# One core, attention and two feed-forward layers: state products of both streams in turns, weight splits of the first tile one step later, duo 0 begun by stream

## The reference

```python
for t in range(S):
    kt, vt, rt, wt = (k[:, :, t], v[:, :, t], r[:, :, t], w[:, :, t])
    cur = np.einsum('bhd,bhe->bhde', u[None] * kt, vt)
    y[:, :, t] = np.einsum('bhd,bhde->bhe', rt, state + cur)
    state = wt[:, :, :, None] * state + np.einsum('bhd,bhe->bhde', kt, vt)
```

## Time and profile before

| | |
|---|---|
| median of 3 runs | 1038.68 us (1038.28 to 1040.86) |
| the profiled execution | 1039.2 us |
| its span, first to last instruction | 1037.2 us |
| PE busy | 1011.8 us (98%) |
| DVE, ACT, POOL busy | 559.3, 289.1, 31.5 us |
| mean granted TensorE clock | 0.997 |

### The profile page before, as it was taken

One profiled execution on the slowest core, in us unless ns is written; L12 is line 12 of the kernel. 1 busy time (PEld: TensorE's weight loads), 2 busy tenths in 40 slices (PEclk: granted clock), 3 DMA queues, 4 the chain that ended last, 5 costly groups with the idle time before them and its releaser, 6 DMA issues.

```text
span 1037.2 us, 29081 instructions
## 1 busy us (share of the span) xinstructions
PE 1011.8 (98%) x12448; PEld 986.6 (95%) x12448; DVE 559.3 (54%) x1170; ACT 289.1 (28%) x604; POOL 31.5 (3%) x29
## 2 busy tenths in 40 slices
PE   4899999999999999999999999999999999999998
PEld 4789999999999999999999999999999999999998
DVE  6576575654655655646542345655455545455454
ACT  3424424224133142241222333222222222222211
POOL 3600100000000000000000000000000000000000
PEclk9989999999999999999999999999999999999999
DMA  7453231301212113011010222110101010101000
GB/s 181 110 147 106 54 101 29 89 25 33 86 52 63 29 52 90 2 52 37 24 48 13 84 84 85 39 46 1 46 1 46 2 45 0 45 0 46 1 24 23
DMA packets 42167, 53.01 MB, mean 51 GB/s; under 512 B 5184, under 2 KB 42048, under 8 KB 42048
## 3 DMA queue, kind: packets, MB, share of 16 engines
q1 hardware_dynamic: 40624, 51.04, 17.3%
q10 hardware_dynamic: 1424, 0.23, 0.2%
HBM read 39.46 MB, written 9.44 MB: 47 GB/s over the span
## 4 chain that ended last, share of the span: by engine, by line
PE 95%; DMA 2%; DVE 1%; issue 1%; SPq 1%; ACT 0%; DVEq 0%; ACTq 0%
PE products L164 17%; PE products L165 16%; PE products L166 16%; PE acc L164 11%; PE acc L166 11%; PE acc L165 11%; PE products L688 6%; PE products L745 2%; PE products L732 1%; PE products L703 1%; DMA w_v<-in_w_dram 1%; PE products L717 1%; PE products L665 1%; DMA stage<-in_w_a_dram 0%; SPq L360 0%
## 5 line engine op out<-in xcount | busy, mean ns | idle before, releaser
L164 PE MATMUL products<-x_parts,weights_hi 128*128 128x384 f32 x576 | 201.4, 350 | 3.1 <-DMA x_parts<-f_y 1.3
L165 PE MATMUL products<-x_parts,weights_hi 128*128 128x384 f32 x576 | 194.6, 338 | 0.0
L166 PE MATMUL products<-x_parts,weights_lo 128*128 128x384 f32 x576 | 194.3, 337 | 0.0
L1207 DVE TENSOR_SCALAR leaky_low<-products,leaky_al 128x384 f32<-128x384 f32 x128 | 79.0, 617 | 169.4 <-PE products L166 169.3
L1067 DVE TENSOR_TENSOR g_sb<-a_g,products 128x384 f32<-128x384 f32 x96 | 53.2, 554 | 203.2 <-issue 141.5
L1154 ACT ACTIVATE leaky_g_hi<-leaky_g_sb 128x384 fp32r<-128x384 f32 x128 | 67.3, 525 | 295.0 <-DVE leaky_g_sb L1212 295.0
L510 ACT ACTIVATE g_hi<-g_sb 128x384 fp32r<-128x384 f32 x96 | 50.3, 524 | 247.0 <-DVE g_sb L1067 247.0
L164 PEld LDWEIGHTS products<-x_parts,weights_hi 128*128 128x128 f32 x576 | 108.5, 188 | 8.1 <-issue 4.6
L165 PEld LDWEIGHTS products<-x_parts,weights_hi 128*128 128x128 f32 x576 | 108.6, 189 | 0.0
L166 PEld LDWEIGHTS products<-x_parts,weights_lo 128*128 128x128 f32 x576 | 108.6, 188 | 0.0
L164 PE MATMUL acc<-g_hi,weights_hi 128*128 128x384 f32 x288 | 97.8, 340 | 2.4 <-DVE g_lo L1073 2.4
(11 more groups left out here) (86 smaller groups left out, 1784.5 us busy)
## 6 DMA issues: line engine op xcount, KB each, us to landing
k_in<-in_k_dram SPq DMA_DIRECT2D x16, 336.0 KB, 4.1
r_in<-in_r_dram SPq DMA_DIRECT2D x16, 336.0 KB, 5.6
stage<-in_w_out_dram SPq DMA_DIRECT2D x14, 384.0 KB, 3.2
w_v<-in_v_dram SPq DMA_DIRECT2D x16, 288.0 KB, 3.2
y_dram<-x_in SPq DMA_DIRECT2D x8, 576.0 KB, 3.0
x_in<-y_dram SPq DMA_DIRECT2D x8, 576.0 KB, 4.5
out_dram<-leaky_out_sb SPq DMA_DIRECT2D x7, 576.0 KB, 3.3
stage<-in_w_dram SPq DMA_DIRECT2D x10, 336.0 KB, 3.9
```

Source lines behind the costliest of these rows:

```text
L164: pe.matmul(out, w_hi, x_hi, start=first, stop=False)
L165: pe.matmul(out, w_hi, x_lo, start=False, stop=False)
L166: return pe.matmul(out, w_lo, x_hi, start=False, stop=last)
L1207: dve.tensor_scalar(self.low[f % 2][:, :], h, 0.0, self.al[:, f:f + 1], ALU.min, ALU.mult).then_inc(self.low_ready, 1)
```

## The change

1. `outputs`: in duos 1 to 7 the weighted values of stream 1 come first, and then the state products of both streams, block by block in turns, uncrossed and then crossed. Before, stream 0's came around the weighted values, then all of stream 1's. Duo 0 keeps one stream after the other.
2. Weights of tile 0: pieces 6 to 10, 12 and 14 are split one step later (`FIRST_NEW`), and ACT does so behind `g_hi` and not ahead of it. Piece 3 is split between the outputs of the two streams of duo 0.
3. Duo 0: the leaf of stream 1 goes into `acc`; PE makes leaf and level 1 of stream 0, then leaf and level 1 of stream 1; DVE steps stream 0's keys for level 2 ahead of stream 1's first step. SP waits for the second `w` before it issues the first three pieces.
4. Duo 1: its `w` is loaded from ACT's queue between the outputs of duo 0, as soon as the weighted values have read `v`, and not from SP's behind the moves; the first steps of its keys and queries stand ahead of step 0 of tile 0 and not in it.

```diff
-HI_AT = [2, 3, 4, 9, 11, 11]
+HI_AT = [2, 3, 4, BEFORE_TILES, 11, 11]
+BETWEEN_OUTPUTS = 3
+FIRST_NEW = [6, 6, 7, 8, 9, 10, 12, 14, 16, 17, 18, 18, 18]
 def new_pieces(f):
-    return range(EARLY + f + max(f - 5, 0) - max(f - 7, 0), EARLY + f + 1 + max(f - 4, 0) - max(f - 6, 0)) if f < 10 else range(0)
+    return range(FIRST_NEW[f], FIRST_NEW[f + 1])
...
-                return (acc[hd], 0) if n == 1 and j == 1 else (products, stream_bank(j, hd))
+                return (acc[hd], 0) if n <= 1 and j == 1 else (products, stream_bank(j, hd))
...
                 load_w(0, 1)
+                sp.wait_ge(w_loaded[1], 16)
                 for piece in range(STAGES):
                     shared.load_piece(sp, piece)
...
-                        if n + 1 < STAGED_FROM:
+                        if 1 < n + 1 < STAGED_FROM:
                             load_w(n + 1, 0)
...
+                def load_first_w(j):
+
+                    act.wait_ge(products_done[j], after(0, 8))
+                    load(act, w_v, w, 1, j, TT, TT, w_loaded[j], into=S * j)
...
                     elif phase == 10:
-                        copy_outputs(n)
+                        copy_outputs(n, 0)
+                        if n == 0:
+                            load_first_w(0)
+                            shared.split_hi(act, BETWEEN_OUTPUTS)
+                            load_first_w(1)
+                        copy_outputs(n, 1)
...
-                    if tile == 0:
-                        for piece in new_pieces(f):
-                            shared.split_hi(act, piece)
                     act.wait_ge(g_ready, g + 1)
                     act.wait_ge(down_done, from0(g - 1))
                     copy(g_hi[f % 2][:, :], g_sb[:, :]).then_inc(g_hi_ready, 1)
+                    if tile == 0:
+                        for piece in new_pieces(f):
+                            shared.split_hi(act, piece)
...
-                    if phase < 3:
+                    if phase >= 3:
+                        pe.wait_ge(merged, merges(n, phase - 2, 1))
+                    elif phase == 2 or n > 1:
                         pe.wait_ge(merged, merges(n, 0, 5 - 2 * phase))
-                    else:
-                        pe.wait_ge(merged, merges(n, phase - 2, 1))
-                    for j in range(2):
+                    for j in streams:
...
                     for c in range(CH):
-                        for hd in range(2):
-                            par = 1 - hd if crossed else hd
...
+                        for j in streams:
+                            for hd in range(2):
+                                par = 1 - hd if crossed else hd
...
                     else:
                         weighted_values(n, 1)
-                        state_products(n, 0, True)
-                    pe.wait_ge(r_stepped[1], 6 * n + 6)
-                    state_products(n, 1, False)
-                    state_products(n, 1, True)
+                        for j in range(2):
+                            pe.wait_ge(r_stepped[j], 6 * n + 6)
+                        state_products(n, (0, 1), False)
+                        state_products(n, (0, 1), True)
...
-                    if phase == 0:
+                    if step == 0:
+                        for j in range(2):
+                            leaf(n, j)
+                            level(n, 1, (j,))
+                    elif phase == 0:
                         leaf(n, 0)
                         leaf(n, 1)
-                    elif 2 <= phase <= 6:
+                    elif 2 <= phase <= 6 and step != 2:
...
-                        if n >= STAGED_FROM:
-                            first_step_k(n, 1)
-                    elif phase == 1 and n > 0:
                         if n == 1:
                             for j in range(2):
                                 first_step_k(n, j)
                                 step_r(n, j, 0)
+                        if n >= STAGED_FROM:
+                            first_step_k(n, 1)
+                    elif phase == 1 and n > 0:
                         products_of_w(n, 0, 2)
...
                 merge_leaf(0, 0)
+                step_k(0, 0, 1)
                 first_step_k(0, 1)
```

More of the change, by code:

```diff
@@ L342, in move_rows, with load @@
                 engine.dma_start(to, f_y[row0 + 16 * q:row0 + 16 * q + 16, 0:S].rearrange("p (h t) -> p h t", h=2)).then_inc(moved[q], 16)
+            def load(engine, tile, source, n, j, at, columns, loaded, rows=ROWS, into=0):
+                first = 4 * (n // 2) + 2 * j
+                engine.dma_start(view(tile, into, [[columns, 2], [1, columns]], rows),
+                                 source[first:first + 2, :, at:at + columns].rearrange("u p s -> p u s")).then_inc(loaded, 16)
             def wait_moved(engine, n):
@@ L357, in _ @@
             def _(sp):
[L358 to L361, removed]
                 def load_w(n, j):
                     if 0 < n < STAGED_FROM:
-                        sp.wait_ge(products_done[j], after(n - 1, 9))
+                        sp.wait_ge(products_done[j], after(n - 1, 8))
                     elif n == STAGED_FROM:
@@ L369, in load_w @@
                         decays_used(n - 1, j)
-                    load(decays_of(n), w, n, j, TT * (n % 2), TT, w_loaded[j], into=S * j)
+                    load(sp, decays_of(n), w, n, j, TT * (n % 2), TT, w_loaded[j], into=S * j)
                 def decays_used(n, j):
@@ L391, in load_v @@
                         sp.wait_ge(products_done[j], after(n - 1, 8))
-                    load(w_v, v, n, j, HALF * E2 * (n % 2), HALF * E2, v_loaded[j], P, into=S * j)
+                    load(sp, w_v, v, n, j, HALF * E2 * (n % 2), HALF * E2, v_loaded[j], P, into=S * j)
                 def move_last_unit(n):
@@ L558, in copy_outputs @@
                     for j, ps, hi, _ in output_parts(n):
-                        act.wait_ge(products_done[j], after(n, 9))
-                        copy(hi, ps).then_inc(copied, 1)
+                        if j == stream:
+                            act.wait_ge(products_done[j], after(n, 9))
+                            copy(hi, ps).then_inc(copied, 1)
+                def load_first_w(j):
+                    act.wait_ge(products_done[j], after(0, 8))
+                    load(act, w_v, w, 1, j, TT, TT, w_loaded[j], into=S * j)
                 def attend(step):
@@ L629, in _ @@
                         attend_late(step_at(g - 1))
+                    act.wait_ge(g_ready, g + 1)
+                    act.wait_ge(down_done, from0(g - 1))
+                    copy(g_hi[f % 2][:, :], g_sb[:, :]).then_inc(g_hi_ready, 1)
                     if tile == 0:
@@ L734, in weighted_values, with state_products @@
                     last.then_inc(products_done[j], 1)
-                def state_products(n, j, crossed):
+                def state_products(n, streams, crossed):
+                    last = {}
                     if crossed:
-                        pe.wait_ge(products_done[j], after(n, 8))
+                        for j in streams:
+                            pe.wait_ge(products_done[j], after(n, 8))
                     for c in range(CH):
-                        for hd in range(2):
-                            par = 1 - hd if crossed else hd
[L743 to L748, removed]
+                        for j in streams:
+                            for hd in range(2):
+                                par = 1 - hd if crossed else hd
+                                b = 2 * HALF * (n % 2) + 2 * (c % HALF) + par
+                                if b > 0:
+                                    last[j] = pe.matmul(view(products, stream_bank(j, par) + BLOCK * c, [[1, BLOCK]], D, 64 * (hd ^ j)),
+                                                        view(state[j], D * (BLOCKS * (c // HALF) + b), [[1, D]], D, 64 * hd),
+                                                        key_blocks(queries_of(n, j), hd, c, par),
+                                                        start=False, stop=True, skip_group_check=True)
@@ L749, in state_products @@
                     if crossed:
-                        last.then_inc(products_done[j], 1)
+                        for j in streams:
+                            last[j].then_inc(products_done[j], 1)
                 def outputs(n):
-                    pe.wait_ge(r_stepped[0], 6 * n + 6)
-                    state_products(n, 0, False)
                     if n == 0:
-                        state_products(n, 0, True)
-                        weighted_values(n, 1)
+                        for j in range(2):
+                            if j == 1:
+                                weighted_values(n, j)
+                            pe.wait_ge(r_stepped[j], 6 * n + 6)
+                            state_products(n, (j,), False)
+                            state_products(n, (j,), True)
@@ L1058, in _ @@
                 for step in range(BEFORE_TILES):
-                    attend_early(step)
```

(2 more changed lines are left out.)

14 lines of the change are left out of this document (6 added, 8 removed).

## The result

The changed kernel takes 1035.6 us in the median of 20 runs (1032.5 to 1038.0), the kernel before 1038.0 in 20 runs beside them: ratio 0.9978 [0.9969, 0.9986], 2.4 us less where 5.9 were forecast. Twelve more runs of it later gave 0.9986 [0.9973, 0.9998], 1.5 us less. The time is inside the range; the size of the gain is wrong.

A forecast was written before the change was run, and what follows sets the result against it. TensorE, busy 98% of the span, bounds the kernel after about 58 us. −6.8 − 1.5 − 0.9 − 2.7 + 3.5 − 0.5 + 3.0 = −5.9 from 1039.2, less 0.5: 1032.8 us, range 1028.8 to 1037.

The forecast's parts named there:

- Part 1: Outputs of duos 1 to 7: state products in turns use all four quarters, 16 ns a record, −6.8 us.
- D: Rival on the outputs: turns give nothing, 27 ns per record whatever the order, 1039.6 us; chance 0.09.
- E: Rival on the state products of duos 1 to 7: each quarter waits for the one before, 1056.5 us; chance 0.06.
- Part 2: Duo 0, before the tiles: the second `w` lands earlier as SP holds weight transfers back, −1.5 us (−0.1 to −2.8).
- the floor of 11: Start: earliest landing of the second `w`, six first loads needing 8 us from 3 us on; ceiling 13.87.
- Part 3: First `down`: `g_hi` goes first, PE waits 1.2 us in place of 2.1, −0.9 us (−2.1 to 0).
- `g_hi` of step 6: Step 6: `g_hi` no longer behind a split that waits for its transfer, PE's wait at 97.90 goes, −0.5 us.
- Part 4: Behind the first `down`, 58.40 to 65.20: no clock drop with the shorter wait, −2.7 us (−3.4 to 0).
- Part 5: Projection of step 6: PE waits +3.5 us for piece 10, low clock behind it +3.0 us (0 to 3.4).
- C: Rival: two low stretches, the first `down` waits as long as before, 1036.4 us, no difference; chance 0.17.

The follow-up runs named there:

- turns alone: The kernel before with only the state products of duos 1 to 7 in turns between the streams: 1030.2 us, ratio 0.9935.
- piece 10 later: The kernel before with only weight pieces 10 to 14 split as the change does: 1042.0 us, ratio 1.0048.
- duo 0 as before: The three edits with duo 0 put back as before the change: 1026.9 us, ratio 0.9899 to the kernel before.
- three edits: The change with piece 10 split in step 4, `w` of duo 1 on SP behind the moves, decays of round 1 behind `g_sb`: 1027.0 us, 0.9909.
- decays ahead: The three edits with the decays of round 1 back ahead of `g_sb`: 1028.1 us, ratio 0.9913 to the kernel before.
- `w` ahead: The three edits with the load of `w` for duo 1 back on ACT's queue ahead of the moves: 1030.3 us, ratio 0.9935.
- duo 0 alone: The kernel before with only the change of duo 0, SP's wait and piece 3's new place included: 1036.5 us, ratio 1.0001.
- three edits again: The three edits run once more without any edit: 1027.4 us, ratio 0.9906 to the kernel before.
- `w` behind the moves: The change with the two loads of `w` for duo 1 on SP again, behind its moves into `x_parts`: 1032.5 us, ratio 0.9958.

## Why the prediction was wrong, point by point

**Part 1, turns (−6.8): right.** Measured −6.7 [−8.2, −5.2] alone, and −7.2 by the traces. Rivals D and E are out.

**Part 2, duo 0 (−1.5): wrong.** With SP's wait the second `w` was there by 10.97, at the floor of 11 that I had set, but the new start is worth 0.0 ± 1.0 us alone. I took the landing of `w` at 13.87 as a property of the kernel before; it was one execution's. In three others with the same start DVE used it at 11.2, 11.6 and 11.1 (turns alone, piece 10 later, duo 0 as before), without SP's wait, so there was little for that wait to save.

**Part 3, the first `down` (−0.9), and `g_hi` of step 6 (−0.5): right in direction, for a mixed reason.** I left 1.2 us of PE's wait there, and it is gone altogether from the change's profile, partly since the projection before it is now slow and late. On the three edits the new table and `g_hi` first are worth 2.7 to 3.1 us. The decays ahead cost 0.4 to 1.1 us, if anything. My reason was wrong: POOL's splits did not hold them. In the change they ran from 47.86 on and the last began at 49.26, when POOL's first split began at 49.29; what they can cost is the wait for `w`, as the run with them ahead shows.

**Part 4, the clock near 58 (−2.7): the step that failed.** I expected no drop ahead of step 6. The stretch did go from 58, and another stood at 47.84. What I left out of the sum, a term at nothing without a reason, is the load of `w` for duo 1, which the change puts on ACT's queue ahead of the moves into `x_parts`. I priced the decays that it serves and never its own 672 KB, which are in transit when the moves are issued. The moves then take 5.4 us to land in the run with `w` ahead and 2.4 in the three edits (medians of one profile each; over all profiles 3.3 to 5.4 with `w` ahead, 2.2 to 3.9 without). The first projection of tile 0 starts between 48.9 and 50.7 in the four profiles with `w` ahead and between 45.6 and 48.0 in the others, and PE's wait of 2.9 to 4.7 us has the low clock in it or right behind it in all four. This costs 2.7 to 3.3 us, measured alone (3.0 ± 1.6 by the means of the six runs with `w` ahead and the eleven of the three edits). The load is not the only way to such a stretch: in four of the ten profiles without `w` ahead (turns alone, duo 0 alone, duo 0 as before, three edits again) PE waits 2.8 to 3.3 us for `x_parts` with the low clock too. Besides, −2.7 was the price of one profile's 6.8 us stretch; over 45 runs the kernel before loses only 1.9 us of clock, so there was less to win. Its place was one execution's as well, as the profile of turns alone shows.

The Trainium skill (DMA: Bandwidth & Descriptors, "Issuing engines are not separate DMA queues") says that transfers started by different engines run on the same 16 DMA engines and interleave. The traces agree: with the two loads on ACT's queue the four moves that SP issues took 5.7 us to land in the median, against 2.4 and 3.4 in the two profiles of the three edits. The other two moves are issued on ACT's queue themselves, so for them these runs do not tell bytes in transit from the queue. By that rule the move to another queue frees nothing when the bytes stand ahead.

**Part 5, piece 10 (+3.5 and +3.0): right in kind, with the clock somewhat too dear.** The wait is 3.3 and its low stretch is there in the trace, 2.7 more. Together 5.8 by the traces, +5.0 to +5.6 by the times alone, 4.3 to 5.1 where it is taken back.

**What the sum becomes.** Measured one at a time: turns −6.7, duo 0 0.0, table and `g_hi` −2.9, `w` ahead +3.0, decays ahead +0.7, piece 10 +5.0, together −0.9, where −2.4 and −1.5 were measured, each term being good to 1 to 2 us, so that the rest of 0.6 to 1.5 says nothing. In the other reckoning, clock lost went from 1.9 to 5.8 and 4.8, 3.6 us more over all 32 runs, where the prediction had −2.7 + 3.0 = +0.3: the 3.3 us between are nearly all of the 3.5 that are missing. (Clock lost inside a wait costs nothing, so this reckoning is an upper bound of the clock's share.) Of the rivals, C (two low stretches, 1036.4) has the right count and nearly the right time, and the wrong place.

**Left open.** Why the wait for `x_parts` differs by 1 us or more between executions of one program, also without `w` ahead, was not tried; nor was whether fewer bytes ahead of the moves would do, or the same loads ahead of them on SP's queue. PE's wait for `x_in` at the end of tile 0 is 0.7 us in the change and 0.2 to 0.8 in the other profiles of versions with the turns and a part of the rest; it is not in the kernel before nor in turns alone, and was not followed up.

## What to carry to other kernels

When a load is moved ahead, price its bytes against every transfer that starts while it is in transit, above all small ones that the next matmul waits for; another queue does not separate them. Take no gain from a landing time that one profile shows: look at the same stretch in a second execution, or at a kernel whose start is the same. And count the clock over many runs (their mean granted clock) beside the waits, since the wait of 3.3 us for piece 10 cost 5.8 in the trace with the clock behind it.

## What the runs showed that was not expected

- Not every wait has a low clock behind it: two of 1.92 and 1.79 us within 7 us had none, one of 1.72 had none, one of 2.79 had one, in the same stretch of nearly the same program. Before the first `down`, one of 2.09 (before) and one of 1.98 (piece 10 later) had one, and one of 1.88 (`w` behind the moves) had none. Those of 2.9 us and more that stand in front of projections all had one in these profiles, also where `w` was not ahead (3.3 us in the turns alone).
- The low stretches of one program vary in number and length from execution to execution: the change's 20 runs have mean clocks of 0.992 to 0.997, those of the kernel before 0.996 to 1.0.
- State products of 48 × 48 in turns over all four quarters take 15 ns a record, and 27 over two.
